# Delta-rule attention, an ELU network and top-2 experts: products of 64 key positions for the diagonal blocks, taken in four copies

## What is computed

```python
k_n = k / (np.linalg.norm(k, axis=-1, keepdims=True) + 1e-06)
for t in range(S):
    y[:, :, t] = einsum('bhd,bhde->bhe', q[:, :, t], state)
    v_old = einsum('bhde,bhd->bhe', state, k_n[:, :, t])
    state += beta[:, :, t, None, None] * einsum('bhd,bhe->bhde', k_n[:, :, t], v[:, :, t] - v_old)
x = y.transpose(0, 2, 1, 3).reshape(B * S, H * D)      # 3072 tokens of 384
x = elu(x @ moe_w_in) @ moe_w_out                      # 384 -> 2048 -> 384
out = top2_of_8_experts(x)                             # noisy gate; relu(x @ w1[e]) @ w2[e], 384 -> 1024 -> 384
```

## Time and profile before

| what | us |
|---|---|
| median of 3 runs (lowest to highest) | 1165.01 (1163.78 to 1166.38) |
| the profiled execution's own time | 1167.03 |
| its span in the trace | 1165.3 |
| PE busy | 1116.0 |
| DVE, ACT, POOL busy | 647.7, 462.6, 355.7 |
| first part (attention), until the first PE work of the second | 275.2 |

### The profile page before, as it was taken

How to read it: one execution, slowest core, us unless ns; L and a number is a source line. 1 busy time by engine, 2 the same in 40 slices (tenths; PEclk the granted TensorE clock), 3 DMA queues, 4 the chain that set the end, 5 groups by cost and what they waited for, 6 DMA issues and landing times.

```text
span 1165.3 us, 29047 instructions
## 1 busy us (share of the span) xinstructions
PE 1116.0 (96%) x11562; PEld 1069.2 (92%) x11562; DVE 647.7 (56%) x1552; ACT 462.6 (40%) x1048; POOL 355.7 (31%) x378
## 2 busy tenths in 40 slices
PE   4898999999999999999999999999999999999996
PEld 3786787888999999999999999999999999999995
DVE  4989787763465646565565657533434343434442
ACT  1236665884333343333333345323333333333331
POOL 5289995541002012020202102322223232322223
PEclk9999999999999999999999999999999999999998
DMA  7544657646996010010101011472424242434221
GB/s 158 126 128 105 166 135 172 164 139 237 366 360 208 25 58 35 27 41 20 41 20 42 22 43 66 172 235 73 170 79 166 86 157 94 147 103 140 61 69 53
DMA packets 82603, 137.30 MB, mean 118 GB/s; under 512 B 11050, under 2 KB 70034, under 8 KB 81466
## 3 DMA queue, kind: packets, MB, share of 16 engines
q1 hardware_dynamic: 68490, 87.97, 25.9%
q0 software_dynamic: 12992, 28.75, 7.7%
q10 hardware_dynamic: 1008, 18.97, 4.4%
HBM read 81.96 MB, written 53.77 MB: 116 GB/s over the span
## 4 chain that ended last, share of the span: by engine, by line
PE 74%; DVE 1%; issue 0%; ACT 0%; POOL 0%; ACTq 0%; POOLq 0%
PE ps_x L1426 18%; PE ps_x L1516 18%; PE ps_h L1415 18%; PE ps_h L1494 17%; PE ps_r L1474 2%; PE ps_r L1465 2%; DVE hg L1834 0%; ACT hg L1624 0%; POOL out_dram L1381 0%; DVE w_parts L1797 0%; PE ps_r L1533 0%; DVE x_raw L1827 0%; PE ps_r L1443 0%; ACT yT_d L1642 0%; PE ps_r L1441 0%
## 5 line engine op out<-in xcount | busy, mean ns | idle before, releaser
L1516 PE MATMUL ps_x<-hg,w_parts 128*128 128x400 f32 x1152 | 230.2, 346 | 0.0
L1426 PE MATMUL ps_x<-w_parts,hg 128*128 128x400 f32 x1152 | 229.7, 345 | 0.0
L1415 PE MATMUL ps_h<-xg,w_parts 128*128 128x384 f32 x1152 | 222.4, 338 | 0.0
L1494 PE MATMUL ps_h<-xg,w_parts 128*128 128x400 f32 x1116 | 220.6, 345 | 1.1 <-DVE w_parts L1797 1.1
L1426 PEld LDWEIGHTS ps_x<-w_parts,hg 128*128 128x128 f32 x1152 | 209.7, 188 | 0.0
L1834 DVE SCALAR_TENSOR_TENSOR hg<-ps_h,hg 128x400 fp32r<-128x400 f32 x128 | 73.6, 575 | 243.1 <-ACT hg L1624 242.6
L1415 PEld LDWEIGHTS ps_h<-xg,w_parts 128*128 128x128 f32 x1152 | 204.0, 188 | 2.5 <-DVE elu_parts L1691 2.5
L1494 PEld LDWEIGHTS ps_h<-xg,w_parts 128*128 128x128 f32 x1116 | 202.7, 188 | 4.0 <-issue 3.1
L1516 PEld LDWEIGHTS ps_x<-hg,w_parts 128*128 128x128 f32 x1152 | 206.1, 188 | 0.0
L1361 POOL DMA_INDIRECT xs_scratch<-x,rows_now x48 | 49.5, 1032 | 393.4 <-DVE rows_now L1771 294.7
L1624 ACT ACTIVATE hg<-ps_h 128x400 fp32r<-128x400 f32 x128 | 64.6, 505 | 256.5 <-PE ps_h L1494 256.5
(11 more groups left out here) (175 smaller groups left out, 1309.8 us busy)
## 6 DMA issues: line engine op xcount, KB each, us to landing
xs_scratch<-pads SPq DMA_DIRECT2D x2, 5502.0 KB, 41.9
x_rows<-xs_scratch SPq DMA_DIRECT2D x17, 614.1 KB
kqT<-in_kqT_dram SPq DMA_DIRECT2D x48, 192.0 KB, 4.0
carried<-in_w_dram ACTq DMA_DIRECT2D x3, 3072.0 KB, 11.2
w_raw<-in_w_dram ACTq DMA_DIRECT2D x3, 3072.0 KB, 11.4
xs_scratch<-pads SPq DMA_DIRECT2D x6, 1375.5 KB, 16.5
out_dram<-pads SPq DMA_DIRECT2D x1, 4800.0 KB, 30.1
xs_scratch<-pads SPq DMA_DIRECT2D x6, 786.0 KB, 9.0
```

What stands on the lines that cost most here:

```text
L1415: mm = nc.tensor.matmul(ps_h[f % 2][:, 0:TB], wi[:, 1 - a, k, f * P:(f + 1) * P], xr[:, b, k, :], start=(i == 0), stop=(i == len(passes) - 1))
L1426: mm = nc.tensor.matmul(ps_x[t][:, 0:DG], act_r[:, f % RING, a, t * P:(t + 1) * P], wo[:, b, f, :], start=(f == 0 and i == 0), stop=(f == ...
L1494: mm = nc.tensor.matmul(ps_h[f % 2][:, 0:TR], w1, xg[:, b, k, :], start=(m == 0), stop=(m == len(passes) - 1))
L1516: mm = nc.tensor.matmul(ps_y[k][:, 0:TR], w2r[i][:, a, s, k * P:(k + 1) * P], hg[:, s % RING, b, :], start=(s == 0 and m == 0), stop=(s == ...
```

## The change

The diagonal blocks now come from products of 64 positions (32 matmuls instead of 64 for each `i`): a 64 x 64 result holds the two wanted 32 x 32 blocks in its corners and two that nobody wants. So `ps_d` has 64 columns for each unit, and each fourth of the rows is copied by itself (`quarter_of`, four copies of 32 x 512 instead of one of 128 x 512, each with its own semaphore). For the first `EARLY_BLOCKS = 4` blocks `ps_d` has two places, and DVE copies two of the four quarters (`take_blocks` on DVE); from the fifth on there is one place and ACT copies all four. Block 0 has keys of its own from `load_kT(0)`, which goes first; `kqT` of chunks 0 and 1 is loaded behind the keys of blocks 0 to 3, and the loads wait for a later `chunk_done`. The first four `products_of_keys` move behind blocks 3 and 4; ACT copies them to `lq` (`take_products`) and POOL masks them there, in place. All masking leaves out the first 32 of 256 columns, which nothing reads. `PREPARED` is 10 instead of 12. The 16 pieces of gate work stand one each behind blocks 5, 6 and 7, three behind 8, 9 and 10, four behind 11. One `keep_clock(256)` is gone. `place(1, s)` stands at the end of m = 2 and 4, `place(2, s)` at the end of m = 6 and 7.

```diff
@@ -59,8 +59,10 @@
...
-PREPARED = 12
+PREPARED = 10
 KEEP_BUSY = 29
+EARLY_BLOCKS = 4
+GATE_WITH = {5: (0,), 6: (1,), 7: (2,), 8: (3, 4, 5), 9: (6, 7, 8), 10: (9, 10, 11), 11: (12, 13, 14, 15)}
...
@@ -125,7 +127,7 @@
...
         ps_y, ps_s = psum[:, 4], psum[:, 5]
-        ps_d = psum[:, 0:2]
+        ps_d = [psum[:, 6 * i:6 * i + 2].rearrange("p h (ca j) -> p h ca j", j=2 * BLK) for i in range(2)]
         ps_wo, ps_gate = psum[:, 6, 0:D], psum[:, 7]
...
@@ -211,6 +214,29 @@
...
+        def blocks_of(i):
+            return ps_d[i % 2 if i < EARLY_BLOCKS else 0]
+        def quarter_of(i, q):
+            to = gram[rows_of(q), i * 2 * H:(i + 1) * 2 * H, :].rearrange("p (ca h) j -> p h ca j", h=2)
+            return to, blocks_of(i)[rows_of(q), :, :, q % 2 * BLK:(q % 2 + 1) * BLK]
+        def kept_keys(n, c, h):
+            pairs = lq[n % KEPT].rearrange("p (g a h) s t -> p g a h (s t)", g=2, h=2)
+            return pairs[:, :, c * QP // 2:(c + 1) * QP // 2, h, BLK:]
+        def keys_made(h):
+            return of_keys(h).rearrange("p g a s t -> p g a (s t)")[..., BLK:]
+        def mask_of_keys():
+            flat = masks[:].rearrange("p g s t -> p g (s t)")[:, :, BLK:]
+            return flat.unsqueeze(2).to_broadcast([P, 2, QP // 2, 2 * P - BLK])
         def heads(h):
...
@@ -228,8 +254,7 @@
...
-            at = 2 * (i - KT_BUFS - 1)
-            return (at, at + 1) if at >= 0 else ()
+            return GATE_WITH.get(i, ())
...
@@ -318,10 +343,8 @@
...
             given = beta_lanes.rearrange("(r n u) x -> r n u x", r=NR, u=H)
+            load_kT(0)
             load_kT(1)
-            for n in range(2):
-                sp.wait_ge(kqT_cleared, n + 1)
-                load_kqT(n)
             sp.dma_start(turned[:, :, half(0)], given[:, :, half(0)]).then_inc(beta_moved, 16)
...
@@ -333,24 +356,28 @@
...
             load_kT(2)
-            for i in range(3, KT_BUFS + 1):
-                sp.wait_ge(chunk_done, i - 2)
-                load_kT(i)
+            load_kT(3)
+            sp.wait_ge(kqT_cleared, 1)
+            sp.wait_ge(chunk_done, 2)
+            load_kqT(0)
             sp.wait_ge(beta_moved, 48)
             sp.dma_start(beta_sb[:].rearrange("p s i -> p (s i)"), beta_turned).then_inc(beta_loaded, 16)
+            sp.wait_ge(chunk_done, 3)
+            load_kT(4)
+            sp.wait_ge(kqT_cleared, 2)
+            sp.wait_ge(chunk_done, 4)
+            load_kqT(1)
             for i in range(KT_BUFS + 1, NIT // 2):
...
-                sp.wait_ge(chunk_done, i - KT_BUFS + 1)
+                sp.wait_ge(chunk_done, i - 1)
                 load_kT(i)
...
                     load_output_weights(f)
-            for f in chunks_with(NIT // 2):
-                load_output_weights(f)
             sp.wait_ge(kqT_cleared, DEEP)
...
@@ -427,6 +454,13 @@
...
+            pool.wait_ge(masks_cleared, 1 + 2 * (NR - 1 + 2))
+            for n in range(2):
+                for c in range(2):
+                    for h in range(2):
+                        pool.wait_ge(grams_taken, (2 * n + c) * 2 + h + 1)
+                        nc.gpsimd.tensor_tensor(kept_keys(n, c, h), kept_keys(n, c, h), mask_of_keys(), ALU.mult
+                                                ).then_inc(masked, 1)
             pool.wait_ge(cleared, len(by_pool))
...
@@ -456,24 +490,19 @@
...
-                if i == 0:
-                    for n in range(2):
-                        pe.wait_ge(kqT_loaded[n], 32)
-                else:
-                    pe.wait_ge(kT_loaded[i % KT_BUFS], (i + KT_BUFS - 1) // KT_BUFS * 32 if i % KT_BUFS else i // KT_BUFS * 32)
-                    pe.wait_ge(blocks_taken, i)
+                pe.wait_ge(kT_loaded[i % KT_BUFS], i // KT_BUFS * 32 + 32)
+                if i == 1:
+                    pe.wait_ge(products_cleared, 1)
+                for q in range(NR):
+                    pe.wait_ge(quarter_taken[q], i if i >= EARLY_BLOCKS else max(i - 1, 0))
                 for ca in range(2 * NP):
                     g, a = ca // QP % NG, ca % QP
-                    for r in range(NR):
-                        to = block_at(g, r)
+                    for r in range(2):
+                        to = (r + g) % 2
                         for h in range(2):
-                            if i == 0:
-                                k_u = kqT[ca // NP][heads(h), g, 0, a, rows_of(r)]
-                            else:
-                                k_u = kT[heads(h), i % KT_BUFS, ca // QP, a, rows_of(r)]
-                            mm = nc.tensor.matmul(ps_d[rows_of(to), h, ca * BLK:(ca + 1) * BLK], k_u, k_u,
-                                                  start=True, stop=True)
+                            k_u = kT[heads(h), i % KT_BUFS, ca // QP, a, r * PADH:(r + 1) * PADH]
+                            mm = nc.tensor.matmul(blocks_of(i)[to * PADH:(to + 1) * PADH, h, ca], k_u, k_u, start=True, stop=True)
                 mm.then_inc(chunk_done, 1)
...
@@ -605,20 +637,21 @@
...
             for i in range(NIT // 2):
-                if i < 4:
-                    products_of_keys(i // 2, i % 2)
                 diagonal_blocks(i)
+                if i == 3:
+                    products_of_keys(0, 0)
+                if i == 4:
+                    for n, c in (0, 1), (1, 0), (1, 1):
+                        products_of_keys(n, c)
                 gate_work(i)
-            gate_work(NIT // 2)
-            pe.wait_ge(blocks_taken, NIT // 2)
+            for q in range(NR):
+                pe.wait_ge(quarter_taken[q], NIT // 2)
             gate_columns(FT1 - 1)
...
             pe.wait_ge(from_lanes, 1)
-            keep_clock(256)
             keep_clock(256)
...
@@ -702,9 +735,9 @@
...
                 act.wait_ge(chunk_done, i + 1)
-                units = gram[:, i * 2 * H:(i + 1) * 2 * H, :].rearrange("p (ca h) j -> p h ca j", h=2)
-                nc.scalar.activation(units, ps_d[:, :, 0:2 * NP * BLK].rearrange("p h (ca j) -> p h ca j", j=BLK),
-                                     ACT.Copy).then_inc(blocks_taken, 1)
+                for q in range(2 if i < EARLY_BLOCKS else NR):
+                    to, blocks = quarter_of(i, q)
+                    nc.scalar.activation(to, blocks, ACT.Copy).then_inc(quarter_taken[q], 1)
...
@@ -742,6 +775,11 @@
...
+            def take_products(n, c):
+                act.wait_ge(grams_done, 2 * n + c + 1)
+                for h in range(2):
+                    nc.scalar.activation(kept_keys(n, c, h), keys_made(h), ACT.Copy).then_inc(grams_taken, 1)
             def take_turned(f):
...
@@ -774,15 +812,17 @@
...
             for i in range(NIT // 2):
+                take_blocks(i)
+                if i == 3:
+                    root_of(0)
+                    take_products(0, 0)
                 if i == 4:
-                    root_of(0)
-                if i == 8:
+                    for n, c in (0, 1), (1, 0), (1, 1):
+                        take_products(n, c)
+                if i == 7:
                     root_of(1)
-                take_blocks(i)
                 for f in chunks_with(i):
                     take_turned(f)
-            for f in chunks_with(NIT // 2):
-                take_turned(f)
             take_gate()
...
@@ -841,10 +881,17 @@
...
         def _(dve):
+            def take_blocks(i):
+                dve.wait_ge(chunk_done, i + 1)
+                for q in range(2, NR):
+                    to, blocks = quarter_of(i, q)
+                    nc.vector.tensor_copy(to, blocks).then_inc(quarter_taken[q], 1)
             def to_set_lanes(g, sets):
...
                 for s in sets:
-                    dve.wait_ge(blocks_taken, (s + 1) * BLK // (2 * H))
+                    for q in range(NR):
+                        dve.wait_ge(quarter_taken[q], (s + 1) * BLK // (2 * H))
                     nc.vector.transpose(lane_a[:, s].rearrange("p i j -> p (i j)"),
...
@@ -924,10 +971,7 @@
...
                 for h in range(2):
-                    to = lq[n % KEPT].rearrange("p (g a h) s t -> p g a h (s t)", g=2, h=2)[:, :, c * QP // 2:(c + 1) * QP // 2, h]
-                    nc.vector.tensor_tensor(to, of_keys(h).rearrange("p g a s t -> p g a (s t)"),
-                                            masks[:].rearrange("p g s t -> p g (s t)").unsqueeze(2).to_broadcast([P, 2, QP // 2, 2 * P]),
-                                            ALU.mult).then_inc(masked, 1)
+                    nc.vector.tensor_tensor(kept_keys(n, c, h), keys_made(h), mask_of_keys(), ALU.mult).then_inc(masked, 1)
...
@@ -961,12 +1005,12 @@
...
             nc.vector.memset(lane_t[0], 0.0).then_inc(zeros_set, 1)
-            dve.wait_ge(masks_cleared, 1 + 2 * (NR - 1 + 2))
-            mask_products(0, 0)
-            mask_products(0, 1)
-            mask_products(1, 0)
-            mask_products(1, 1)
-            to_set_lanes(0, (0, 1))
+            take_blocks(0)
+            take_blocks(1)
+            to_set_lanes(0, (0,))
+            take_blocks(2)
```

(15 more changed lines are left out.)

9 lines of the change are left out of this document (6 added, 3 removed).

## The result

| | kernel before | changed kernel |
|---|---|---|
| median of the runs side by side, us | 1165.6 (1163.8 to 1166.4, 4 runs) | 1171.0 (1169.7 to 1172.4, 4 runs) |
| ratio, 95% interval | 1 | 1.0052 (1.0038 to 1.0065) |
| a second measurement (20 and 11 runs) | 1166.5 | 1172.6, ratio 1.0048 (1.0035 to 1.0061) |
| the profiled execution, us (its span) | 1167.03 (1165.3) | 1169.66 (1167.8) |
| first k load issued, us | 73.41 | 77.87 |

The kernel is 0.5% slower: the medians differ by 5.4 us and, in the second measurement, by 6.1; 0.48% would be 5.6. The two profiled executions differ by only 2.5 us in their spans. Their second parts are equally long (1165.3 - 275.17 = 890.1 and 1167.8 - 277.63 = 890.2), so the whole difference of these two executions arises before 277.63.

What follows compares the result with a forecast made beforehand. Gate piece 15, through SP's loads of v and then POOL, was taken to bound the kernel: +4.6 - 0.3 = +4.3 us on 1167.03 gives 1171.3, or 1169.3 on the median's footing; range 1161.5 to 1174.

Steps and rivals of the forecast that it cites:

- What bounds it: Opening into loop: late gate piece 15 delays SP's v loads, then POOL, making the seventh pair 4.6 us late.
- A block and its copies: Diagonal blocks on PE and ACT: block 1.8 us plus 0.2, four quarter copies 2.45; three-piece period 8.8 against 5.2.
- The opening: Blocks 0 to 3 and DVE's norms: first column starts at 23.5, 9.7 us earlier than 33.17.
- Then the gain stops: Blocks 4 to 7: DVE waits for block 7 from 35.0 to 41.3; placing starts at 71.5, 3.5 us earlier.
- The loop: m = 0 to 6: shorter masks save DVE 1.5 us, placing about 1 for PE; POOL, 4.6 late, binds from m = 5.
- Placing set 4: End of m = 6: DVE waits 2 us for POOL, yet the placing gives back up to 0.6, taken as 0.3.
- The sum: Whole kernel: +4.6 - 0.3 = +4.3 us on 1167.03, giving 1171.3, or 1169.3 on the median's footing.
- The clock did not rise in the gate work: Rival in the gate work, chance 0.12: TensorE's clock rises, pieces take 1.0 us, time 1160.5.
- Weight loads cost nothing: Rival in blocks 5 to 11, chance 0.10: weight loads not hidden, +1.8 us each, 1182 at most, 1176 half hidden.
- The quarter copies did not overlap: ACT's four copies: forecast without overlap, 2.45 us; the skill's overlap would make about 2.2, the sum some 1.7 less.
- The chain was not shorter than summed: Rival in the gate chain, chance 0.25: copies of 0.5 or PE's pauses hidden take 2.8 off, 1166.5.
- `keep_clock` one shorter: Before the loop, within the forecast's case: clock not raised, m = 0 pays 2.7 us, the end hardly moves.

Runs made afterwards that it cites:

- e1: Changed kernel with v of chunks 2 and 3 loaded ahead of the wait for gate piece 15: 1167.8 us, ratio to before 1.0008.
- e9: Kernel before, with SP also waiting for ACT's copy of the gate before loading k, so k and v come later: 1170.0 us, ratio 1.0025.
- e5: Changed kernel, ACT taking the first turned piece between quarter copies in blocks 8 to 11, root of group 1 behind piece 2: ratio to before 0.9999.
- e7: Changed kernel with POOL's eight masks held back until VectorE has scaled group 0: 1172.0 us, one execution only.
- e4: Changed kernel with the placings of the third and fifth set back before residuals (a, 2) of m = 3 and m = 7: ratio to before 1.0062.
- e8: Kernel before with only VectorE's masks shortened to 448 of 512 elements: ratio to before 0.9985.
- e11: Changed kernel with only the first placing of group 2 back at m = 7: ratio to before 1.0045.
- e12: The changed kernel again, nothing else, measured in the same call as e11: ratio to before 1.0048.
- e2: Kernel before with only v of chunks 2 and 3 loaded early: 1165.0 us, ratio to before 0.9991.
- e3: Changed kernel with blocks 4 to 11 again as products of 32 positions and one ACT copy: 1169.9 us, ratio to before 1.0026.
- e6: Changed kernel with the edits of e5 and the early v loads of e1 together: 1162.9 us, ratio to before 0.9971.

## Why the prediction was right

Forecast 1169.3 and slower by over 0.2%; measured 1171.0, inside the range. Step by step:

- **What bounds it.** Right: e1 moves `v` alone, e9 `v` and a `k` that nobody waits for, and the time follows; e5 moves piece 15 and gets the loss back. The rows show 2.27 us of DVE's waiting in m = 5 and 2.00 at the end of m = 6, the two places named.
- **A block and its copies.** Forecast 1.8 + 0.2 and four copies in 2.45; measured 1.96 to 1.99 and 2.43. VectorE's two quarters took 1.42 instead of 1.24. The period of 8.8 was 8.87, TensorE's idle time of 1.2 was 1.24, the first k load forecast at 78.0 came at 77.87, the first solve forecast at 83.7 at 83.76.
- **The opening.** Here a step failed: "the second transposition ends at 17.8 and the first column starts 5.7 later, 23.5". The transposition ended at 17.84; the column came at 28.02. I had taken 5.7 from the earlier trace rows and cost POOL's eight masks at nothing ("end by 30 and are hidden"); they end by 30.9, but several of DVE's norm steps, and the two products behind them, were stretched beside them, from 0.22 to between 1.0 and 1.2 and from 2.36 to 4.13. Both sides use SBUF only. e7 takes the masks away from there and has 23.70. It cost nothing in the end, as the next step says: DVE waits for block 7 anyway. That a step 4.5 us off left the forecast standing is luck.
- **Then the gain stops.** Right: DVE was released by block 7 (ACT L740), its copies ended at 40.64 (forecast 41.2), and placing started at 71.17 (71.5).
- **The loop.** Forecast: TensorE only about 1 late at m = 4, POOL 4.6 late, binding from m = 5. Measured: 0.3 to 0.9 late at the seventh and eighth outputs, POOL 3.8 late (the k and v issues took 11.0 us instead of 11.8). That DVE saves 1.5 by masks (24 times 0.07 is 1.7) and about 1 by the placing fits e4's 1.5 for the placing and e8's 1.7 (0 to 3.5) for the masks; the single sizes are no better known.
- **Placing set 4.** Forecast from 196.4 after 2 us of waiting, and residuals (a, 2) at 201.8; measured 195.69 after 2.00, and 201.62. That it costs nothing fits e11 and e12, within some 1.5 us.
- **The sum** was +4.3, the medians say +5.4 and, again, +6.1. What is missing is 1 to 2 us, and it was not found. Against POOL's lateness as measured, 3.8 instead of the forecast 4.6, 1.6 to 2.3 us stand in no row. So the path is shown, the full size only in part explained. The spans give only 2.5. A part of that gap can be seen: TensorE paused twice for 1.18 us for instructions in the profiled execution of before, at 127.60 and 224.49, and the second of these stands behind POOL's last elimination, where nothing waits it away: the changed kernel is 3.2 late at the 17th output and 2.2 at the 18th. The changed kernel's execution has in the loop only pauses of 0.50 and 0.58, at 147.89 and 162.71. For the executions without a profile nobody can say where such pauses fell.
- **The rivals.** The clock did not rise in the gate work: L524's weight loads take 332 to 338 ns up to 79.8, 1.2 GHz. Weight loads cost nothing: the block took what streaming alone was forecast to take, 1.96 to 1.99 us. By the Trainium skill (TensorE: Matmul & The Clock Gate, Part 3) they overlap only where the row group differs. I had read half of them as exposed, an estimate of 2.9 us a block, and the measurement decides against that reading. It need not be against the rule: the block's inner loop changes the row group with every matmul, and no run here tells the two apart. The quarter copies did not overlap: 2.43 for four and 1.20 for two, of 0.57 to 0.59 each. ACT's copies of products do: two of 0.54 take 0.98 (18.41), an overlap of 0.10, about what the Trainium skill (ScalarE: Activation LUTs, "What ACT_TABLE_LOAD costs") gives for back-to-back ACTIVATEs. The chain was not shorter than summed.
- **`keep_clock` one shorter.** The first solve took 1.50 us (0.87 in the kernel before), so m = 0 began at the lower clock. But the count of these matmuls doesn't decide it: e2, with the old ten, also has 1.50, and e3, with eight, 0.87.

## What to carry to other kernels

Before a piece of work is split into several instructions on an in-order engine, look at what is queued behind it and who waits for that: here not ACT's 1.8 us more per block but the one copy behind them cost the time, and moving that copy up among them, with the root behind piece 2, gave it back. An engine that is early by 4 us is worth nothing until the latest of the chains that meet is shorter; follow each signal on to all its users (here SP's order of loads, and through it POOL), since the costliest path may leave the stage altogether. And a load that waits only because it stands behind another in SP's program can be moved for nothing.

## What the runs showed of the hardware

- VectorE instructions that only touch SBUF were stretched by up to one GpSimd product beside them: 128 x 64 from 0.22 to 1.04 us, the two of 128 x 1024 from 2.36 to 4.13. The columns, which take one input from PSUM (0.60 for 414 elements), were not, with the same products beside them in e7. Two of GpSimd's products grew as well, from 1.1 to 1.53 and 2.12. The Trainium skill (SBUF — State Buffer, "Who interferes with whom") says that a VectorE instruction with two SBUF inputs contends with a GpSimd instruction that reads SBUF, over a port pair that both share under an exclusive lock. These rows agree with it: a step of 0.22 that starts at 19.33, beside a product of 1.1 begun at 19.10, ends at 20.37, 0.1 after that product's end (20.28).
- A copy of 32 rows x 512 from PSUM takes 0.71 us on VectorE (two in 1.42) and 0.60 on ScalarE (two in 1.20), as much as 128 rows x 512 there.
- In 12 of the 14 traces the granted clock is shown as 1.00 for the whole of the first 100 us, while a weight load of 128 x 128 takes 333 ns until 79.8 and 189 later. e12, the same kernel as the change, shows it as 0.50 from 33 to 84, with the same 333 ns. So the durations tell the clock of the gate work (1.2 GHz), and a 1.00 in the column there doesn't.
- Pauses of GpSimd of 2.8 to 4.9 us in which it waits for nothing shown fall at different places in different kernels, each time ahead of a scaling of values: at 200.61 in the change (4.04), where nobody waits, but at 133.17 in e1 (4.50) and 127.25 in e6 (4.82).
